# Soft mixture of experts between attention and a gated layer: the token softmax in two parts, and weight loads cut and laid out anew

## The reference, cut to what matters

```python
def _moe_ref(x, phi, w1, w2):              # x: 2304 tokens x 512, phi: 512 x 32 slots
    logits = x @ phi
    d = logits - logits.max(0, keepdims=True)      # softmax over the tokens, per slot
    d = np.exp(d)
    d /= d.sum(0, keepdims=True) + 1e-09
    slot_input = (d.T @ x).reshape(8, 4, D)        # 8 experts, 4 slots each
    for e in range(8):
        h = np.maximum(slot_input[e] @ w1[e], 0.0) # w1[e]: 512 x 1024
        slot_out[e] = h @ w2[e]                    # w2[e]: 1024 x 512
    c = logits - logits.max(1, keepdims=True)      # softmax over the slots, per token
    c = np.exp(c)
    c /= c.sum(1, keepdims=True) + 1e-09
    return c @ slot_out.reshape(32, D)
```

## Time and profile before

| | |
|---|---|
| median of 3 runs | 797.98 us (796.89 to 799.02) |
| the profiled execution's own time | 796.09 us |
| its span, first to last instruction | 794.3 us |
| outside the span | 1.8 us |
| granted TensorE clock | 0.998 of full |
| PE busy / DVE / ACT | 98% / 59% / 58% |
| chain of work that ended last | PE 89%, SP queue 4%, DMA 3% |
| HBM read, written | 71.37 MB, 4.72 MB |

### The profile page before, as it was taken

One profiled execution on the slowest core, in us unless ns is written; L12 is line 12 of the kernel. 1 busy time (PEld: TensorE's weight loads), 2 busy tenths in 40 slices (PEclk: granted clock), 3 DMA queues, 4 the chain that ended last, 5 costly groups with the idle time before them and its releaser, 6 DMA issues.

```text
span 794.3 us, 16113 instructions
## 1 busy us (share of the span) xinstructions
PE 777.4 (98%) x5255; PEld 581.0 (73%) x5255; DVE 465.2 (59%) x895; ACT 461.8 (58%) x871; POOL 182.0 (23%) x244
## 2 busy tenths in 40 slices
PE   7999999999999999999999999999988999999998
PEld 7777777777777777777777777667324788888886
DVE  6767667666676666766666666654414545454443
ACT  5767676766767676767676676653104644343433
POOL 5351431513315233152241421000003420000000
PEclk9999999999999999999999999999999999999999
DMA  8539746374473653836538335949999001010101
GB/s 228 130 80 282 211 120 161 80 177 100 108 177 76 163 110 98 192 72 152 119 89 208 73 77 131 339 135 360 347 392 401 10 1 54 0 54 1 54 40 40
DMA packets 83030, 112.01 MB, mean 141 GB/s; under 512 B 45360, under 2 KB 47408, under 8 KB 82480
## 3 DMA queue, kind: packets, MB, share of 16 engines
q1 hardware_dynamic: 82832, 111.24, 49.3%
q10 hardware_dynamic: 160, 0.26, 0.1%
HBM read 71.37 MB, written 4.72 MB: 96 GB/s over the span
## 4 chain that ended last, share of the span: by engine, by line
PE 89%; SPq 4%; DMA 3%; POOL 2%; DVE 1%; issue 1%; ACT 0%; POOLq 0%; DVEq 0%; ACTq 0%
PE banks L521 23%; PE banks L584 20%; PE banks L617 19%; PE banks L1617 18%; SPq L1398 2%; PE banks L1541 2%; DMA weights<-in_moe_w 2%; PE banks L1545 2%; PE banks L1063 1%; DMA q_in<-in_q 1%; PE banks L1117 1%; PE banks L1082 1%; PE banks L1515 0%; PE banks L1468 0%; SPq L322 0%
## 5 line engine op out<-in xcount | busy, mean ns | idle before, releaser
L584 PE MATMUL banks<-k_stack,q_stack 128*128 128x384 f32 x960 | 274.8, 376 | 2.5 <-DVE q_stack L801 2.0
L772 ACT COPY pt<-banks 128x384 f32<-128x384 f32 x288 | 138.3, 480 | 152.9 <-PE banks L521 152.8
L521 PE MATMUL banks<-ident,probs 128*128 128x128 f32 x1296 | 219.6, 278 | 0.4 <-ACT probs L744 0.3
L521 PEld LDWEIGHTS banks<-ident,probs 128*128 128x128 f32 x1296 | 156.5, 140 | 67.7 <-issue 42.0
L744 ACT ACTIVATE probs<-banks,neg_max 128x1152 f32<-128x1152 f32 x144 | 175.9, 1222 | 7.4 <-DVE neg_max L841 3.0
L617 PE MATMUL banks<-pt,v_in 128*64 128x320 f32 (+1 forms) x1152 | 167.3, 417 | 0.9 <-ACT o_t L759 0.9
L584 PEld LDWEIGHTS banks<-k_stack,q_stack 128*128 128x128 f32 x960 | 147.4, 191 | 3.4 <-ACT k_stack L388 2.2
L837 DVE TENSOR_REDUCE row_max<-banks 128x1 f32<-128x384 f32 x144 | 80.1, 556 | 117.0 <-PE banks L584 115.4
L830 DVE TENSOR_REDUCE row_max<-banks 128x1 f32<-128x768 f32 x144 | 136.7, 949 | 1.7 <-PE banks L584 1.1
L617 PEld LDWEIGHTS banks<-pt,v_in 128*64 128x64 f32 x1152 | 72.0, 136 | 58.2 <-issue 25.9
L892 DVE COPY pt<-banks 128x384 f32<-128x384 f32 x144 | 80.3, 558 | 37.0 <-PE banks L521 34.3
(11 more groups left out here) (188 smaller groups left out, 663.3 us busy)
## 6 DMA issues: line engine op xcount, KB each, us to landing
weights<-in_moe_w SPq DMA_DIRECT2D x7, 2048.0 KB, 11.4
v_in<-in_v SPq DMA_DIRECT2D x16, 576.0 KB, 4.0
k_in<-in_k SPq DMA_DIRECT2D x30, 288.0 KB, 4.9
k_stack<-k_hi SPq DMA_DIRECT2D x30, 288.0 KB, 3.6
k_stack<-k_lo SPq DMA_DIRECT2D x30, 288.0 KB, 3.5
q_in<-in_q SPq DMA_DIRECT2D x14, 512.0 KB, 4.9
slots_of_four<-in_moe_w SPq DMA_DIRECT2D x12, 512.0 KB, 10.8
q_stack<-q_hi SPq DMA_DIRECT2D x30, 144.0 KB, 3.3
```

The costliest lines, as they stand in the source:

```text
L521: last = nc.tensor.transpose(tbank[:, bank, cols], src, ident[0:rows, 0:rows])
L584: last = nc.tensor.matmul(scores[:, bank, 0:CH], q_stack[at.par][:, h, order, cols], k_stack[at.par][:, h, keys], start=(x == 0), stop=(x ...
L772: nc.scalar.copy(pt_out(at, e), pt_from(at, e)).then_inc(out_by_act, 1)
```

## The change

Three parts.

1. The token softmax is split by tiles in two parts, `SOON` (tiles 0, 1, 2: 384 columns) and `LATE` (tiles 3, 4: 192 columns). Each has its own PSUM bank for logits (`lt_soon`, `lt_late`), its own maximum, exponential, sum and PSUM bank for the weighted tokens (`z_soon`, `z_late`). `peak`, `factor`, `coef` and the like have two columns. `fold_f` and both `keep_busy` matmuls are gone; the sums are brought together by one ACT instruction with a scale, and two DVE instructions that multiply, add and write `z_sum`. The tail's transposed tokens have a place of their own, `xt_tail`, in the second half of `xt[0]`.
2. The first three quarters of `w1_third`, which were one load of 1.5 MiB behind `lt_step` 5, are three loads of 0.5 MiB behind `lt_step` 3, 4 and 5. The fourth quarter stays behind `slots_done`.
3. Every w2 is read in another order of its rows: partition p of a half n holds the rows 512 n + 4 p to 512 n + 4 p + 3. One contiguous run is 8 KB in the loads of whole experts and 4 KB in the loads of a quarter of an expert, in place of 2 KB. To match, the transposes of `hid` take every fourth feature.

```diff
-        sp.dma_start(mem.w2_last[:], mem.w2_v[3]).then_inc(mem.w2_last_in, 16)
+        sp.dma_start(mem.w2_last[:, :, :].rearrange("p (n f) d -> p n (f d)", n=2), mem.w2_v[3]).then_inc(mem.w2_last_in, 16)
...
+    SOON, LATE = range(0, 3), range(3, NI)
...
-        sp.wait_ge(lt_step, NI)
-        sp.dma_start(w1_next[2][:, 0:3, :], mem.w1_v[4:7, :, 2, :].rearrange("e p f -> p e f")).then_inc(w1_in[2], 16)
+        for r, tile in ((0, NF - 2), (2, NF - 1), (1, NF)):
+            sp.wait_ge(lt_step, tile + 1)
+            sp.dma_start(w1_next[2][:, r, :], mem.w1_v[4 + r, :, 2, :]).then_inc(w1_in[2], 16)
...
+        def exp_transposes(tiles, bank):
+            for m, i in enumerate(tiles):
+                last = nc.tensor.transpose(banks[0:rows_of(i), bank, P * m:P * m + P],
+                                           exp_t[:, P * i:P * i + rows_of(i)], ident[:])
+            last.then_inc(e_ready, 1)
...
+        pe.wait_ge(shares_done, 1)
+        exp_transposes(SOON, 0)
         logits(NF)
-        keep_busy()
...
+        pe.wait_ge(e_out_a, 1)
+        slot_sums(0, z_soon)
         pe.wait_ge(peak_spread, 1)
...
+        slot_sums(1, z_soon).then_inc(z_step, 1)
+        pe.wait_ge(shares_done, 2)
+        exp_transposes(LATE, 3)
+        pe.wait_ge(weight_done, 1)
+        nc.tensor.matmul(total_ps, same_slot[:], weight[:], start=True, stop=True).then_inc(total_ready, 1)
+        slot_sums(2, z_soon).then_inc(z_ready, 1)
+        pe.wait_ge(e_out_v, 1)
+        for i in LATE:
+            last = slot_sums(i, z_late)
         last.then_inc(z_ready, 1)
...
-        nc.scalar.activation(exp_t[:], lt_ps, ACT.Exp, bias=minus_peak[:, 0:1], accum_out=exp_sum[:]).then_inc(shares_done, 1)
+        nc.scalar.activation(exp_t[:, 0:P * len(SOON)], lt_soon, ACT.Exp, bias=minus_peak[:, 0:1],
+                             accum_out=exp_sum[:, 0:1]).then_inc(shares_done, 1)
...
-        for half in range(2):
-            at = slice(2 * P * half, 2 * P * half + 2 * P)
-            nc.scalar.copy(z_sum[:, at], z_ps[:, at]).then_inc(z_out, 1)
+        nc.scalar.activation(z_sum[:], z_soon, ACT.Copy, scale=coef[:, 0:1]).then_inc(z_scaled, 1)
...
-        nc.vector.tensor_scalar(fold_f[:], fold[:], coef[:, 0:1], None, ALU.mult).then_inc(fold_done, 1)
...
+        dve.wait_ge(z_ready, 2)
+        dve.wait_ge(z_scaled, 1)
+        for half in range(2):
+            cols = slice(2 * P * half, 2 * P * half + 2 * P)
+            nc.vector.scalar_tensor_tensor(z_sum[:, cols], z_late[:, cols], coef[:, 1:2], z_sum[:, cols],
+                                           op0=ALU.mult, op1=ALU.add).then_inc(z_out, 1)
...
-                sp.dma_start(w2_next[n][:, r, :].rearrange("p (f d) -> p f d", f=2),
-                             mem.w2_v[4 + r, :, 2 * n:2 * n + 2, :]).then_inc(w2_in[n], 16)
+                sp.dma_start(w2_next[n][:, r, :], mem.w2_v[4 + r, :, n // 2, 2 * DM * (n % 2):2 * DM * (n % 2) + 2 * DM]
+                             ).then_inc(w2_in[n], 16)
...
                 for f in range(4):
                     last = nc.tensor.transpose(t_ps[:, n, P * f:P * f + P],
-                                               hid[:, P * (4 * n + f):P * (4 * n + f) + P], ident[:])
+                                               hid[:, 4 * P * n:4 * P * n + 4 * P].rearrange("q (p f) -> q f p", f=4)[:, f, :],
+                                               ident[:])
...
-        w2_v = moe_w2.rearrange("e (f p) d -> e p f d", p=P)
+        w2_v = moe_w2.rearrange("e (n p f) d -> e p n (f d)", n=2, p=P)
```

127 lines of the change are left out of this document (64 added, 63 removed).

## The result

The changed kernel takes 793.69 us, median of 7 runs (792.01 to 795.80), and the kernel before 797.96 in the 7 runs beside them (796.40 to 799.02): ratio 0.9954 [0.9940, 0.9969]. Timed again on another occasion it took 793.19 (8 runs, 792.43 to 795.99) against 797.27 (31 runs): 0.9949 [0.9932, 0.9966]. The forecast was 794.3. The ratio is worked out over all runs of both kernels and is not the quotient of the two medians (0.9947 in the first set): by the ratio the gain is 3.7 us (2.5 to 4.8) the first time and 4.1 (2.7 to 5.4) the second, by the medians 4.3 and 4.1.

A forecast was written before the change was run, and what follows sets the result against it. The later of the last w2 landing and PE's arrival before the last second-layer matmuls was taken as the bound. Idle DMA 2.2 plus run size 1.4 gave 3.6 us off the median 797.98, so 794.3 us, range 792.3 to 796.9.

The forecast's parts named there:

- What bounds the kernel: Before the second group's last sixteen second-layer matmuls: the later of last w2 landing (595.4) and PE's arrival (592.75) sets the end.
- S: Split token softmax: how much earlier slots_done comes, 2.1 us, with PE's sums ending at 557.6 and slot_in at 559.4.
- The cover on DVE: DVE's work before its slot_in instruction is through at 557.5, hidden behind PE's sums ending at 557.7, by only 0.2 us.
- D, idle DMA (2.2): Loads around 550 to 559: earlier quarters and w_second fill idle DMA time, so the last w2 lands 2.2 us earlier.
- D, size of a run (1.4): Group 1's w2 loads: longer runs raise 388 GB/s to 415, landing 1.4 us earlier; bounds 0 and 1.5.
- the rival without an effect: w2 loads: run size changes nothing, last w2 lands 2.2 us earlier at 593.2, time 795.8; chance 0.12.
- Stragglers (0): End of w2 loading: last piece lands some 3.4 us after w2 is nearly through; left unchanged, 0, could shrink by at most 3.4.
- Strided loads (0.3): Transposes of hid taking every fourth column: 0.3 us later PE arrival (590.95), covered by the DMA wait.
- The granted clock (nothing): PE idling without keep_busy: clock stays at 1.00, as through 2.65 us idle before, so no cost.
- Sum: PE at 590.95, last w2 at 591.8: PE still waits 0.8 us, gain 3.6, median 794.3 us.
- the signs named beforehand: Wait 0.8 us; sums 557.7; slot_in 559.4; w_second 554.4; DMA share near 1 from 550; w2 415 GB/s; hid loads 141 to 190 ns.
- The chance given to a gain of over 0.3%: Whole kernel faster by over 0.3%: 0.78, from the forecast, the PE-bound case and half the dear strides, less the spread.

The follow-up runs named there:

- 6: The changed kernel with four filler matmuls that nothing reads ahead of the wait for the last w2: 795.21 us, ratio 0.9974.
- 7: The changed kernel with w1's third part as one load again and four filler matmuls ahead of the last w2 wait: 794.92 us, ratio 0.9968.
- 3: The changed kernel with the old w2 layout, so split softmax and quarters only: 795.01 us, ratio 0.9974.
- 2: The kernel before with the split softmax alone, one 1.5 MiB load and old w2 layout: 794.84 us, ratio 0.9979.
- 5: The changed kernel timed once more, without an edit, with a second profile: 793.19 us, ratio 0.9949.
- 4: The changed kernel without the quarters, w1's third part as one 1.5 MiB load behind the last logits: 793.10 us, ratio 0.9956.
- 1: The kernel before with the new w2 layout and its strided transposes alone: 796.17 us, ratio 0.9995.
- 9: The kernel before with the w2 layout alone, as in 1, on another chip: 796.94 us, ratio 0.9994.
- 8: 4 with the w_gv loads held back until w2's last piece has landed: 795.06 us, ratio 0.9971.
- 11: 4 with two filler matmuls that nothing reads ahead of the wait for the last w2: 793.20 us, ratio 0.9950.
- 12: 4 once more, unchanged, as the reference beside 9 to 11: 792.93 us, ratio 0.9956.
- 10: 4 with each quarter of the second group's w2 as one 2 MiB load in place of four of 0.5 MiB: 792.45 us, ratio 0.9941.

## Why the prediction was right, and where its steps were off

**What bounds the kernel.** Right. In both profiles of the changed kernel, and in every other experiment but 6 and 7, the last sixteen second-layer matmuls wait for the last w2. With four fillers the wait is gone and the time is set by PE.

**S.** 1.96 to 2.0 measured, 2.1 forecast, and 1.96 again in every profile of the split; the sums end at 557.6, forecast 557.6 to 557.7. `w_second` is issued at 554.38, forecast 554.35. Building it from start-to-start times of the old trace, in the order of the new program, was enough. The cover on DVE, hidden by 0.2 by my count, was hidden by 0.3.

**D, idle DMA (2.2).** The split alone gives 1.7 to 2.4 us in the timed runs, so about what S gives (2.0) is all that came of the term. The step that failed is the quarters: they were to move bytes into the gap while the last logits run, and they do, but two experiments beside their twins without them (3 and 2; 5 and 4) show no gain: 795.01 against 794.84, 793.19 against 793.10 (less than 1 us would not show). What took the gain is in the windows: in the last 6 us ahead of the first first-layer matmul 274 to 345 GB/s with quarters, 393 to 408 with one load. The quarters were to be through near 554.7; the last, issued at 552.0, landed at 556.9. `w_second` goes out 5.45 us ahead of the first first-layer matmul with the quarters (554.38, 559.83) and without them (553.24, 558.69), and lands 9.9 us after its issue in the one and 8.8 in the other (9.5 to 10.1 in the four profiles with quarters, 8.8 to 9.1 in the seven without); in the kernel before it took 7.0. By 5 us behind that matmul as many bytes have moved with the quarters as without (experiment 4). I had counted time at the full rate, not bytes. Why the rate is poor behind the quarters no run shows. The sum's reading of the earlier trace rows has a slip as well: 1.77 us is what the engines idled from 556 to 559, not what they were busy (0.41 of 3 us is 1.23).

**D, size of a run (1.4).** The mechanism is right: 388 GB/s became 408 to 413 from 577 to 590 in every kernel with the new layout, and stayed at 387 or 388 in those without it (before, 2 and 3). That decides between the forecast and the rival without an effect, which the rule of the Trainium skill (DMA: Bandwidth & Descriptors, Specifications), line rate from 512 B up, would have given: the trace disagrees with it here, 2 KB against 4 KB runs. The size is not settled. The windows show half of the term: from 565 to 577 the layout gave nothing on top of the split (395 and 393), so 0.7 us, not 1.4. The timed runs show more on top of the split, 1.7 us (4 beside 2) and 1.8 (5 beside 3), and 1.3 in both pairs among the runs that kept their clock (0.999 or more, see below: 793.90 and 792.62, 794.14 and 792.86). These are few runs. Alone it was worth 0.3 to 0.5 us of reach, and 0.4 and 0.5 us by the ratios of 1 and 9, whose intervals end at 1.5 and 1.8. Whether it gives more behind the split than alone they do not settle. The gain of the first group's loads, which I had set at nothing, was nothing. Why the rate gains only in the second window is not settled. From 9 to 12 us behind the first first-layer matmul single microseconds fall to 225 to 311 GB/s in 4, 5, 7, 8, 9, 11 and 12. In 2 and 3, with the old layout, in 10, with loads of 2 MiB, and in the first profile of the changed kernel none is under 387. No run shows the cause of these dips.

**Stragglers (0).** I left them as they were, and said that nothing shows what they hang on. In experiment 8 they are DMA engines that end one after another, the last of them alone for 1.2 us. They are no constant: over all profiles the reach runs from 32.0 to 33.8 us where the DMA sets it, and one and the same kernel has 33.7 and 32.0. That is as much as any of my terms, and a single profile can't tell such terms apart. What makes an engine late stays open.

**Strided loads (0.3).** 209 ns in place of 141, half as much again: above the third that I took from DVE, far below twice. Eight transposes pass in 1.53 us, in the kernel before in 1.44, so 0.09 a group and 0.18 in all. It never showed in the end, as the DMA wait covered it: PE came to the wait at 590.91 in the first profile, forecast 590.95.

**The granted clock (nothing).** This was a wrong step that did not turn the result. I argued that it had stayed at 1.00 through 2.65 us of idle PE. In the profile of before it did; in the first profile of the changed kernel 2.60 us of idle brought it to half, and so did 2.13, 2.59 and 2.26 us in experiments 2, 3 and 8. The price, by the time from the last sixteen matmuls to the loop, is 1.3 us in the first profile and in 2 and 3. It held through 2.17 us in experiment 1 and 1.97 in 9, and through every shorter wait (0.94 to 1.86). So a wait of 2.1 to 2.65 us goes either way, from run to run. The profile of before lists a mean clock of 0.998 even so, and the reason is elsewhere:

```profile
10.00:12.00 2.00, 2.00 (x11) 1.97 (x10) 1.75 (x4) 0.87 (x2) 1.85 (x5) 0.50 0.87 266
```

At the start of the program PE idled 2.02 us, and the clock fell; the profile of 7 has the same behind 2.46 us, the other twelve, with 1.77 us or less at that place, do not. So a run's mean clock does not say where it fell. The timed runs bear the price out only roughly. Each lists its mean granted clock: of the kernel before, in the three sets, 24 runs had 0.999 or more (medians 795.65, 796.31 and 796.41) and 58 had 0.998 or less (797.54, 797.73 and 797.94). Of the changed kernel 9 had the higher clock (792.85 and 792.86) and 6 the lower (794.94 and 794.65). Among runs of the higher clock the gain is 3.45 us in the second set (796.31 to 792.86), close to the 3.6 of the forecast, which had no clock in it; the measured 4.1 between the medians may hold also that fewer runs lose their clock, though by these means it could be lost at the start as well. In the profiles the clock fell only behind the longer waits, those with a late landing, so the 2 us between the two kinds of runs are not the clock's alone. With the two fillers of 11 the long runs did not come: none of 6, against 2 of 7 beside it. But 10, without fillers, had none in 6 either, so that is no proof.

**Sum.** Gain 3.6 or 3.7 forecast (797.98 less 3.6 is 794.4, not 794.3), 4.3 and 4.1 measured between the medians, 3.7 and 4.1 by the ratios, with 794.3 for 793.7 and 793.2. It came out close partly by luck: the quarters gave nothing, and the two profiles have the landing 1.9 and 3.8 us earlier, where the forecast has 3.6. Of the signs named beforehand the sums' end, `slot_in`, `w_second` and the w2 rate came; the DMA share near 1 from 550 on (0.80 and 0.87 from 550 to 553, 0.77 and 0.92 from 553 to 559) and the `hid` loads of at most 190 ns (209) did not, and the wait of 0.8 us was 2.60 in one profile and 0.94 in the other. How much the straggle and the clock each give to the median was not measured. The chance given to a gain of over 0.3% does not follow from its parts either: 0.52, 0.18 and half of 0.14 are 0.77, and something had to come off for the spread, but 0.78 was written.

## What to carry to other kernels

Where PE ends on a DMA wait, move what lies ahead of the loads first (the split gave most here, and what it gives PE was worked out to 0.15 us from start-to-start times), then make the runs of a load longer; cutting a load into pieces to start it earlier cost the loads behind it here as much as it gained, so count bytes landed by a point, not issues. A wait of some 2 us ahead of dense matmuls costs more than itself when the clock falls behind it (1.3 us here), and the two profiles of one kernel differ by 3.2 us of span: take a second one before a term of 1 us is read off, and count windows from an instruction that both have, not from the start of the program.

## What the runs showed of the hardware

- With nothing else queued, the sixteen DMA engines ended an 8 MiB series of loads one after another; the last worked alone for 1.2 us, and from 592 to 594 the rate was 27 GB/s at a share of 0.07 (experiment 8).
- In the 6 us ahead of the first first-layer matmul, three loads of 0.5 MiB, issued 1 to 2 us apart, and the 2 MiB behind them ran at 274 to 345 GB/s in four profiles; one load of 1.5 MiB and the same 2 MiB at 393 to 408 in seven. From 565 to 577, loads of 2 MiB in place of 0.5 MiB ran at 412 against 391 and 393.
- Runs of 2 KB: 387 or 388 GB/s in three profiles; of 4 KB: 408 to 413 in eleven, from 577 to 590.
- Loads of 128x128 fp32 into the array with a step of 16 bytes: 209 ns against 141 without a step.
- Behind 2.1 to 2.65 us without work ahead of the last w2, PE's granted clock fell to 1.2 GHz in four profiles and stayed at 2.4 GHz in two; at the start of the program it fell behind 2.02 and 2.46 us in two.
